# Routing of the first expert layer, moved from a phase of its own into the attention loop

## What is computed

```python
for t in range(S):                      # B=4, H=8, S=768, D=48
    y[:, :, t] = einsum(r[t], state + (u * k[t]) x v[t])
    state = w[t][:, None] * state + k[t] x v[t]
x = y as [3072 tokens, 384]
# layer 1: xn = x/(|x|+1e-6), en = emb/(|emb|+1e-6)
logits = xn @ en.T / tau;  e = argmax(logits);  gate = softmax(logits)[e]
x = gate * relu(x @ w1[e]) @ w2[e]      # 384 -> 1024 -> 384
# layer 2: the same with logits = x @ w_gate, and a second factor sigmoid(x @ w_output_gate)[e]
```

## Time and profile before

| | us |
|---|---|
| median of 3 runs (lowest, highest) | 946.03 (944.97, 949.33) |
| the profiled execution: its time | 947.32 |
| its span, first to last instruction | 945.6 |
| mean granted TensorE clock (share of full) | 0.916 |
| PE / DVE / ACT / POOL busy | 775.7 / 569.5 / 392.2 / 196.1 |

### The profile page before, as it was taken

How to read it: one execution, slowest core, us unless ns; L and a number is a source line. 1 busy time by engine, 2 the same in 40 slices (tenths; PEclk the granted TensorE clock), 3 DMA queues, 4 the chain that set the end, 5 groups by cost and what they waited for, 6 DMA issues and landing times.

```text
span 945.6 us, 20223 instructions
## 1 busy us (share of the span) xinstructions
PE 775.7 (82%) x4774; PEld 678.1 (72%) x4775; DVE 569.5 (60%) x1437; ACT 392.2 (41%) x768; POOL 196.1 (21%) x218
## 2 busy tenths in 40 slices
PE   0686877667780199999999999992999999999995
PEld 0575766556530188989888898881899999999994
DVE  4999999999364035574747556654444535434631
ACT  2344344443470034453535545530443534434531
POOL 5544444445005400000100000000001010101010
PEclk9979788897895599999999999996899999999998
DMA  4453534455174302441414335332344424333310
GB/s 110 126 138 113 148 102 138 116 145 209 35 234 169 118 17 68 132 157 50 160 43 160 100 100 165 101 100 86 101 140 142 136 71 167 109 101 104 104 37 30
DMA packets 46726, 108.30 MB, mean 115 GB/s; under 512 B 6601, under 2 KB 25616, under 8 KB 46704
## 3 DMA queue, kind: packets, MB, share of 16 engines
q1 hardware_dynamic: 29632, 67.91, 23.2%
q10 hardware_dynamic: 11952, 25.88, 9.2%
q0 software_dynamic: 5120, 14.26, 4.1%
HBM read 90.60 MB, written 19.01 MB: 116 GB/s over the span
## 4 chain that ended last, share of the span: by engine, by line
PE 63%; DVE 18%; issue 10%; ACT 3%; ACTq 2%; POOL 1%; SPq 1%; DMA 1%; DVEq 0%; POOLq 0%
PE bank L1087 16%; PE bank L1113 15%; PE bank L1121 8%; PE bank L1092 8%; DVE Q L643 6%; PE bank L1102 5%; DVE SF L653 4%; PE bank L1076 2%; PE bank L1054 2%; PE bank L1029 2%; ACT w_hi L506 2%; DVE Kb L657 2%; DVE St L675 1%; DVE Rq L648 1%; PE bank L1012 1%
## 5 line engine op out<-in xcount | busy, mean ns | idle before, releaser
L735 DVE TENSOR_TENSOR w_lo<-raw,w_hi 128x1024 f32 (+1 forms) x96 | 112.1, 1221 | 66.0 <-ACT w_hi L506 66.0
L1113 PE MATMUL bank<-w_hi,hT_hi 128*128 x440 | 150.3, 342 | 1.0 <-ACT hT_hi L565 0.5
L1113 PE MATMUL bank<-w_lo,hT_hi 128*128 x440 | 147.8, 336 | 0.0
L1087 PE MATMUL bank<-w_hi,xT_hi 128*128 x330 | 138.9, 421 | 1.6 <-ACT xT_hi L556 1.6
L1087 PE MATMUL bank<-w_lo,xT_hi 128*128 x330 | 131.9, 400 | 0.0
L560 ACT ACTIVATE hs<-bank 128x512 f32<-128x512 f32 x110 | 65.1, 592 | 114.1 <-PE bank L1092 106.8
L506 ACT ACTIVATE w_hi<-raw 128x1024 f32 (+1 forms) x96 | 94.8, 1049 | 38.6 <-issue 38.6
L1092 PE MATMUL bank<-w_hi,xT_lo 128*128 x330 | 95.2, 397 | 0.0
L565 ACT ACTIVATE hT_hi<-bank 128x512 fp32r<-128x512 f32 x110 | 59.7, 595 | 76.1 <-PE bank L1102 76.1
L1121 PE MATMUL bank<-w_hi,hT_lo 128*128 x440 | 90.9, 348 | 0.0
L414 POOL DMA_INDIRECT sorted<-yrow,slot x28 | 27.2, 972 | 300.8 <-DVE yrow L853 300.8
(11 more groups left out here) (194 smaller groups left out, 1320.8 us busy)
## 6 DMA issues: line engine op xcount, KB each, us to landing
raw<-wall_in SPq DMA_DIRECT2D x96, 512.0 KB, 3.9
rkv<-rkv_src ACTq DMA_DIRECT2D x24, 576.0 KB, 5.3
xin<-sorted ACTq DMA_DIRECT2D x59, 194.0 KB
rk<-rk_in SPq DMA_DIRECT2D x48, 192.0 KB, 3.7
wb<-w_in SPq DMA_DIRECT2D x48, 96.0 KB, 3.4
sorted<-padrow SPq DMA_DIRECT2D x16, 194.0 KB, 1.9
sorted<-yrow,slot POOLq DMA_INDIRECT x28, 2.6
out<-ybuf,toki POOLq DMA_INDIRECT x28, 2.6
```

What stands on the lines that cost most here:

```text
L735: v.tensor_tensor(w_lo[:, slot, cols], raw[:, q], w_hi[:, slot, cols].bitcast(F32), ALU.subtract).then_inc(w_split, 1)
L1087: pe.matmul(bank[n][:, :], xT_hi[:, k, :], w[:, bass.ds(slot, 1), cols].rearrange("p o n -> p (o n)"), start=(k == 0 and w is w_hi), stop= ...
L1113: pe.matmul(bank[2][:, 0:DM], hT_hi[:, j, :], w[:, bass.ds(slot, 1), W2 + j * DM:W2 + (j + 1) * DM].rearrange("p o n -> p (o n)"), start=( ...
```

## The change

- The unit loop is unrolled on PE, DVE, ACT and POOL (`each_unit`); SP's loop stays.
- `rows` holds two chunks by turns instead of all 24 units.
- PE, in step u, begins with three transposes of the output of unit u-1 (`transpose_x1`, into bank 2; it waits for `x_ready`), then does `attend(u+1)`, then the three small router products of unit u-1 (`logits1`, into bank 3). All `attend`s share banks 0 and 1. In the last chunk only its first unit does this.
- DVE routes chunk c-1 inside chunk c: `choose1` in unit b=1 (norms, logits, one-hot), `place1` in unit b=3 (gate, slots); both stand between `pre` and the wait for `su_done`. PE ranks the chunk (`ranks1`, 13 small products) at the end of unit b=2. ACT takes the roots at the end of unit b=0 and the exponentials at the end of b=1. POOL scatters the four units of chunk c-1 at the end of unit b=3.
- `logits1` has two waits: in unit b=1 for `lgc`, which `choose1` raises when it has read the logits, and in unit b=3 for `rread`, which `place1` raises when it has read the ranks.
- `sum8` carries the next free slot of each expert from chunk to chunk. The slots no longer need the totals of all tokens, since each expert has a region of its own.
- After the loop the last chunk is routed by a loop of one pass (`passes` comes from the flag; the general path would take seven). `padi` and the tables follow it on DVE, after the branch over the general path. SP's `pads(0)` comes ahead of the raw loads.
- Before the first expert layer only expert 0 is split (ACT: half ahead of the last routing, half after; DVE after the tables); expert 1 is split in the tile loop.

```diff
-            with eng.Fori(0, NCHUNK - 1) as c:
+            for c in range(NCHUNK):
                 for b in range(B):
-                    step(c, B * c + b, b, B * c + b + ahead, (b + ahead) % B)
...
@@ GpSimd
+            def scatter(c, q):
+                gp.wait_ge(rts[0]["slots"], c + 1)
+                part(gp)
+                for b in range(B):
+                    gp.indirect_dma_start(
...
                 if nu is not None:
                     masks(nu, nb)
+                if b == B - 1 and c > 0:
+                    scatter(c - 1, (c - 1) % 2)
...
@@ ScalarE
+                if u > 0 and not (last_chunk and b > 0):
+                    copy_x((b - 1) % B, 2, u)
...
+                if c > 0 and b == 0:
+                    roots(c - 1)
+                if c > 0 and b == 1:
+                    exps1(c - 1)
...
+            for q in SOON:
+                split_hi(0, 0, q)
+            act.wait_ge(fl_ready, 1)
+            passes = act.value_load(flag[0:1, 0:1], min_val=1, max_val=NCHUNK + 1)
+            with act.Fori(0, passes) as j:
+                act.wait_ge(rts[0]["ready"], j + 1)
+                act.activation(r4[:, 0, :], ssq[:, UNITS - B:UNITS], ACT.Sqrt).then_inc(rts[0]["root"], 1)
+                for b in range(B):
+                    copy_x(b, XBANK[b], B * (j + NCHUNK - 1) + b + 1)
+                exps1(j + NCHUNK - 1)
+            for q in LATE:
+                split_hi(0, 0, q)
...
@@ VectorE, step
                 if nu is not None:
                     pre(nu, nb)
+                if c > 0 and b == 1:
+                    choose1(c - 1, c - 1)
+                if c > 0 and b == 3:
+                    place1(c - 1, (c - 1) % 2)
 
                 v.wait_ge(su_done, u + 1)
...
+                if c > 1 and b == 0:
+                    v.wait_ge(rts[0]["sorted"], 16 * B * (c - 1))
+                if b == 0:
+                    v.tensor_scalar(rows[:, c % 2, :, TOK], tokbase[:, :], float(c * C), None, ALU.add)
...
+            def choose1(n, c):
...
+                v.wait_ge(rt["root"], n + 1)
+                step(1, v.tensor_scalar(safe, norm, 1e-30, None, ALU.max))
...
+                step(6, v.reciprocal(scale, t5))
+                v.wait_ge(rt["lg"], B * n + B)
+                v.tensor_tensor(zs, bank[3][:, 0:B * E].rearrange("p (b e) -> p b e", e=E), bcast_inner(scale, E), ALU.mult).then_inc(rt["lgc"], 1)
...
+                v.tensor_tensor(oh4[:, :, :], bcast_mid(iota8[:, :], B), bcast_inner(first, E), ALU.is_equal).then_inc(rt["oh"], 1)
+
+            def place1(n, q):
...
+                v.wait_ge(rt["cnt"], n + 1)
+                v.tensor_tensor(z4[:, 2], bank[3][:, 2 * B * E:3 * B * E].rearrange("p (b e) -> p b e", e=E), oh4[:, :, :], ALU.mult)\
+                 .then_inc(rt["rread"], 1)
+                v.tensor_copy(sum8[:, :], bank[3][:, 4 * B * E:4 * B * E + E]).then_inc(rt["rread"], 1)
...
+                v.tensor_copy(slot4[:, q], at).then_inc(rt["slots"], 1)
...
@@ TensorE
             def step(c, u, b, nu, nb):
                 par = b % 2
+                logits_due = u > 0 and not (c == NCHUNK - 1 and b > 0)
+                if logits_due:
+                    pe.wait_ge(x_ready, u + 1)
+                    transpose_x1((c - (b == 0)) % 2, (b - 1) % B, 2, u - 1)
                 if nu is not None:
                     attend(nu, nb)
+                if logits_due:
+                    if b == 1 and c > 0:
+                        pe.wait_ge(r1s["lgc"], c)
+                    if b == 3 and c > 0:
+                        pe.wait_ge(r1s["rread"], 2 * c)
+                    logits1((b - 1) % B, u - 1)
...
+                if c > 0 and b == 2:
+                    ranks1(c - 1)
```

More of the change, by code:

```diff
@@ L88, in build @@
         padrow = sb("padrow", [P, ROW])
-        rows = sb("rows", [P, UNITS, ROW])
+        rows = sb("rows", [P, 2, B, ROW])
+        xT1 = sb("xT1", [P, B, KC, P])
+        raw = sb("raw", [P, RAWS, RAWC])
         wbad = sb("wbad", [P, UNITS])
@@ L225, in each_unit @@
                 first(b, b)
-            with eng.Fori(0, NCHUNK - 1) as c:
+            for c in range(NCHUNK):
                 for b in range(B):
-                    step(c, B * c + b, b, B * c + b + ahead, (b + ahead) % B)
-            for b in range(B):
-                u = B * (NCHUNK - 1) + b
-                step(NCHUNK - 1, u, b, u + ahead if b + ahead < B else None, (b + ahead) % B)
+                    u = B * c + b
+                    step(c, u, b, u + ahead if u + ahead < UNITS else None, (b + ahead) % B)
         SOON, LATE = range(3), range(3, RAWS)
@@ L305, in _ @@
             sp.wait_ge(fl_ready, 1)
-            ok = sp.value_load(flag[0:1, 0:1], min_val=0, max_val=1)
-            with sp.If(ok < 1):
+            passes = sp.value_load(flag[0:1, 0:1], min_val=1, max_val=NCHUNK + 1)
+            with sp.If(passes > 1):
                 for g in range(4 * B):
@@ L397, in step @@
                     masks(nu, nb)
+                if b == B - 1 and c > 0:
+                    scatter(c - 1, (c - 1) % 2)
             each_unit(gp, 1, first, step)
[L401 to L406, removed]
+            gp.wait_ge(fl_ready, 1)
+            passes = gp.value_load(flag[0:1, 0:1], min_val=1, max_val=NCHUNK + 1)
+            with gp.Fori(0, passes) as j:
+                scatter(j + NCHUNK - 1, 1)
             gp.sem_inc(row_free, 1)
@@ L694, in _ @@
             v.wait_ge(fl_ps, 1)
-            v.tensor_scalar(flag[0:1, 0:1], bank[7][0:1, 0:1], 0.0, None, ALU.is_equal).then_inc(fl_ready, 1)
-            v.wait_ge(fl_ready, 1)
-            ok = v.value_load(flag[0:1, 0:1], min_val=0, max_val=1)
-            with v.If(ok < 1):
+            link(v.tensor_scalar(flagp[0:1, 3:4], bank[7][0:1, 0:1], 0.0, -float(NCHUNK), ALU.is_equal, ALU.mult))
+            v.tensor_scalar(flag[0:1, 0:1], flagp[0:1, 3:4], float(NCHUNK + 1), None, ALU.add).then_inc(fl_ready, 1)
+            v.sem_inc(rt["ready"], 1)
+            choose1(NCHUNK - 1, NCHUNK - 1)
+            place1(NCHUNK - 1, 1)
+            passes = v.value_load(flag[0:1, 0:1], min_val=1, max_val=NCHUNK + 1)
+            with v.If(passes > 1):
                 v.memset(gst[:, :, :], 0.0).then_inc(g_step, 1)
@@ L855, in _ @@
             tables(0)
+            for q in range(RAWS):
+                split_lo(0, 0, q)
             link(v.memset(ybuf[:, :], 0.0))
```

261 lines of the change are left out of this document (129 added, 132 removed).

## The result

| | us |
|---|---|
| the changed kernel, median of 4 runs (lowest, highest) | 981.11 (977.86, 985.08) |
| the kernel before, 4 runs beside them | 946.31 (944.97, 949.33) |
| ratio, 95% interval | 1.0365 [1.0314, 1.0416] |
| profiled execution of the changed kernel: time, span | 977.86, 976.1 |
| mean granted TensorE clock (before 0.916) | 0.894 |

The account below looks back on a forecast made before the run. DVE was taken to pace the attention loop, PE the expert layers. Terms 52.8 + 3.8 + 1 - 47.7 + 0.6 = +10.5 on 947.3 profiled gave 957.8, less 1.3 to the median: 956.5 us, 8-in-10 range 937 to 972.

Parts of the forecast that it names:

- The hold of PE: Waits in logits1 hold products DVE needs: b=1 6.8, b=3 6.2 us over; 52.8 with TOK step, chunks 1 to 4.
- Rival (a): PE, held in units b=1 and b=3, recovers at once: -7.9, 938 us; chance 0.13.
- Two table loads of 1.28 per chunk fall into units with idle time: ACT's two added table loads of 1.28 us per chunk hide in the loop, ACT being busy 43%.
- `ranks1` "delays a burst of b=3 that then waits for `rread` anyway": PE's 13 rank products ending b=2, up to 5.6 us, only delay a burst that waits anyway.
- rival (c): Plain units stall too, PE at the lower clock after its 2.5 us of idle: +14, 970 us; chance 0.15.
- Unrolling at 0: Unrolling the unit loop saves no time; fetching longer code could cost 0 to 5 us, taken as 0.
- rival (d): POOL's scatter, locked out by DVE, holds dv and so rows beyond 11 us of cover: +28, 985 us; chance 0.04.
- The stretch behind the loop: From last rows to the first tile's transposes: shrinks from 81.5 to 33.8 us, -47.7, to within 5.
- Rival (e): Path after the loop longer, by register-count loops on four engines or late raw loads: +8, 965 us; chance 0.04.
- Layer 1: Expert layer 1 splits expert 1 in the tile loop, one more switch: +0.6 us.
- DVE's own work 4.6 per chunk: DVE's added steps in the loop: choose1 3.1, place1 1.3, TOK step 0.2 us; 23 us over five chunks.
- Rival (b): The hold costs nothing, waits being met when PE gets there; only DVE's steps count: -23, 923 us; chance 0.09.

Follow-up runs that it names:

- experiment 1: The changed kernel with logits1 and its two waits moved to the end of PE's step, behind the transposes of YT: 943.77 us, ratio 0.998.
- experiment 5: As experiment 1, with the transposes of x and ACT's copy of xT also behind what the unit's output needs: 942.89 us, ratio 0.9946.
- experiment 6: As experiment 5, with padi written ahead of DVE's branch and raw loads waiting for the first tile: 938.37 us, ratio 0.9916; again 939.65, 0.9931.
- experiment 7: As experiment 6, with logits1 of b=1 and its wait for lgc moved to the end of b=2: 939.04 us, ratio 0.9905.
- experiment 8: As experiment 6, with two scatters at the end of b=3, one in the next b=0, one in b=1: 938.15 us, ratio 0.9905.
- experiment 4: The changed kernel with expert 1's six raw weight loads waiting until the first sorted tile has landed: 980.8 us.
- experiment 2: As experiment 1, but the wait for rread in b=3 stays behind attend: 950.47 us, ratio 1.005.
- experiment 3: The changed kernel with 16 unread 128 x 128 products on PE ahead of each of the two waits: 973.22 us, ratio 1.0291.

## Why the prediction was right and wrong, point by point

The mechanism was right: PE is held behind `attend`, and that makes the kernel slower. The sum was 20 us short on the profiled span (30.5 for 10.5), and no single term has it. The steps that failed are two things taken as hidden in the loop, the table load in b=2 (4.8 us) and the ranks of the last chunk (some 4.5), and the stretch behind the loop, 41.3 us for 33.8. Besides, the hold came out 4 us larger and layer 1 3 us; other parts of the loop came out some 4 us smaller.

- **The hold of PE, the term that decides: right in place and nature, nearly in size.** Over a unit of 9.3, forecast 4 x (6.8 + 6.2) = 52 us, measured 4 x (7.7 + 6.4) = 56. Of that, experiment 1 takes away 4 x (4.8 + 4.4) = 37; the rest is mostly DVE's own steps, which 6.8 and 6.2 held too. b=1 was 0.9 too low, half of it ahead of the logits and half behind. PE went on at R + 8.5 on average (7.5 to 10.1) and not R + 8.0: in three of the four units a DVE operation or two ahead of the read of the logits took 0.7 to 0.85 us longer each while POOL ran the two products ruk. The longest has Kb at 1.50 us, where the earlier trace rows have 0.69, and a small step at 0.95 (134.35, 135.77; POOL 134.31 to 136.70). And the three logits products held St x Rq back by 1.3 us for the 0.9 that I took.
- **Rival (a), PE recovers at once: out.** In all four held units b=1 St x Rq took 2.05 to 2.06 us behind 5.9 to 8.4 us of idle, the lower level.
- **"Two table loads of 1.28 per chunk fall into units with idle time": the first step that failed.** ACT is busy 43% of the loop, but the exponential's load stands directly ahead of the copy of xT that PE waits for behind `attend`: b=2 took 10.5 us, not 9.3, 4.8 us over the loop. In each of the four units PE waited 1.5 to 1.8 us for that copy, and the products behind it fell to the lower level (granted clock 0.50 from 98.2 on in the first), where I had said that these units "come right after a held unit and start fast": they did start fast. Experiment 1 brought b=2 back to 9.6 (9.55), but it moved the wait for xT and the hold together; no run moved the table load alone. I had asked how busy ACT is, and not what stands behind the load in its queue.
- **`ranks1` "delays a burst of b=3 that then waits for `rread` anyway": right in chunks 1 to 4, not in the last, the second step that failed.** There PE sets the pace (units of 5.65 and 4.12 us before); the 13 products at 302.76 to 305.73 stand ahead of unit 23's products, whose unit took 8.6 us for 4.1 (302.96 to 311.58). That this is the ranks' doing is read from the order of the rows; no run moved them.
- **Units b=0 and b=2 without a stall, rival (c):** b=0 right (9.1); (c), PE slow from its own 2.5 us of idle, is out, for b=2's lateness begins with ACT's. Two bursts of the kernel before that the earlier trace rows don't show lie on this border: after 2.59 and 2.11 us of idle (75.49, 178.09) they started fast and still took 6.4 us to their last transposes, so "after 2.26 us or less the burst started fast" holds for the start only; and ahead of the ten bursts that I counted one started slow after 1.90 us (30.10, 2.08 us).
- **Unrolling at 0: nothing against it.** Every idle time of DVE that the profile lists between 60 and 285 us ends with a release by PE or by a load. The bound of 5 us stood on no row, and no run tests it alone.
- **POOL's scatter, rival (d):** the 24 scatters took 0.967, 0.972 and 1.163 us (least, median, most), as before; they weren't locked out. But the 11 us of cover, 2 without the hold, asked only when `dv` would be late. Behind an unheld PE the price was DVE's operations made slower, 1.5 to 2.1 us in each b=0 and b=1 together (experiments 1 and 5 to 8, against 21.9).
- **The stretch behind the loop: "to within 5" was too bold, the third failed step; 7.5 over, three terms.** Logits T + 10.9 for 8.4: 12 small products that I hid under ACT's copies run at the lower clock level (granted 0.50), 5.13 us. Ranks 5.7 us for the 4 that I took between my own bounds of 2.7 and 5.6, at a granted clock of 0.50 too; in the last chunk the same 13 products took 2.97 us at 1.00 (302.76 to 305.73). The tile's load 6.1 us for 2.4, among six raw loads that had waited for the same pads: experiment 4 takes back 3.7 of it. The branch was right (3.63 for 4.0), pads too (8.43 for 8.65). Rival (e) named two causes, register loops and raw loads; of them only the raw loads came.
- **Layer 1: +3.4 for 0.6.** The first three tiles account for 1.3 (353.45 to 383.52, 30.1 us, where the kernel before took 28.7), with the raw loads still under way; the rest I could not place. In experiment 1's profile the same code took 334.3 us, +0.5, in experiments 2, 3 and 5 336.9 to 337.2. So 3 us come and go from one execution to the next, and whether 0.6 was wrong stays open.
- **"DVE's own work 4.6 per chunk": fits.** Experiment 6 has a chunk of 43.1 us in both profiles where the kernel before had 37.0: 4.6, and 1.5 of operations made slower.
- **Faster and slower cases.** Rival (b), "the hold costs nothing", had 923 us. With an order of instructions in which it does cost nothing the kernel takes 942.9, 0.995 of the time before (experiment 5), and 0.992 with the pads ahead of the branch. Among what (b) lacks are the 7.5 us behind the loop, 1.5 per chunk on DVE, and the last chunk (36.9 us in experiment 5, 28.3 before).

The range was too narrow because small misses of one sign (a queue's neighbour, the tail, three terms behind the loop, layer 1) were taken as independent. Most have one thing in common: each was priced as if PE's clock and the queues around it were as in the kernel before.

## What to carry to other kernels

Work moved into a loop is priced by what stands behind its waits on each in-order engine: a wait for the bounding engine put ahead of products that this engine needs made 37 us here, and the same wait behind them nothing that the runs show. So ask for each added wait, and each added table load, what the next instruction in that queue is and who is waiting for it, not how idle the engine is on average. Where a serial stretch is shortened, take small products behind an idle TensorE at the lower clock level, and look at which transfers the same event releases together.

## What the runs showed of the hardware

- The clock can fall in a row of small products in which PE is never idle. In the changed kernel PE runs ranks from 156.70 to 160.04 and transposes to 160.78; the granted clock is 1.00 up to 158.4 and 0.50 from 160.0, and the `attend` right behind takes 2.08 us, the lower level. It doesn't always: behind the ranks of the other three chunks `attend` took 1.16 (106.67, 211.76, 263.54), the upper level. In the first unit shown of experiment 3, 2.2 us of idle behind 128 x 128 products left the upper one in force, in the second 2.1 us didn't for long. The rows don't tell what decides.

```profile
159.47 0.57 PE L1076 MATMUL bank<-sum,top 128*128 128x8 f32 x2
159.90 0.88 PE L1055 MATMUL bank<-ident,rows 128*128 128x128 f32 x3
160.71 2.08 PE L993 MATMUL bank<-Rq,Kb 64*128 64x128 f32 x16
```

- DVE operations with two operands in SBUF, the on-chip memory, are slowed by POOL operations that read SBUF, one by one: the four scans of Q took 1.36 us in experiment 7 with only scatters on POOL (197.23), 1.95 beside dv (188.04, experiment 6), 2.73 beside dv and a mask (187.66, experiment 7) and 4.53 beside a row of four (157.40, experiment 1). The Trainium skill (SBUF — State Buffer, "SBUF: two separate sides") says that for such a pair the shared port is an exclusive lock for a whole instruction; the trace agrees, with 0.6 to 0.8 us for each POOL operation of 0.7 to 1.0 us; a single scan, 0.42 us alone, took up to 1.84 (157.40). A few small operations with one operand were slowed as well: a step of `choose1` took 1.01 us for 0.17 beside ruk (84.05).
- A second gap that ends with no release follows the branch: 3.63 us before `padi` and 2.34 before the next operation (337.42), where the kernel before shows one of 3.99. In experiment 6, with `padi` ahead of the branch, one gap of 3.53 is left (300.62). What fills them, the trace doesn't say.
- Six raw loads of 512 KB, their issue begun 2.9 us ahead of a tile's load of 194 KB, stretch it from 2.5 to 6.1 us, issue to transposes (experiment 4).
